# Attention of a routed two-stage MLP kernel: scores from split float32r halves, P*V with V stationary, logits from the transposed output

## What is computed

```python
# attention: q, k, v of shape (B=2, H=8, S=768, D=64); block = 32, window = 16
k_sum = k.reshape(B, H, nb, block, D).max(axis=3)
v_sum = v.reshape(B, H, nb, block, D).mean(axis=3)
scores_l = scale * q @ k.T           # only where abs(i - j) < 16, else -1e9
scores_s = scale * q @ k_sum.T + np.log(block)
a = softmax(concat([scores_l, scores_s]))       # the sum gets 1e-9
x = a @ concat([v, v_sum])           # then 1536 tokens of 512
# experts: E=8, F=1024, tau=0.1
logits = (x / (norm(x) + 1e-6)) @ en.T / tau
out = gate * (np.maximum(x @ w1[e], 0) @ w2[e])  # e = argmax(logits)
# dense: d_ff = 2048
h = out @ w_in
g = (a0 + a1*h + a2*h**2 + a3*h**3) / (1 + abs(b0)*abs(h) + abs(b1)*h**2 + 1e-6)
result = g @ w_out
```

## Time and profile before

| | before |
|---|---|
| time of three runs, median (lowest to highest) | 886.83 us (883.63 to 887.01) |
| span of the profiled execution | 909.4 us |
| the profiled execution's own time outside the span | not given apart |
| PE, PEld busy | 776.2 us (85%), 641.1 us (71%) |
| DVE, ACT, POOL busy | 505.2 us (56%), 410.6 us (45%), 92.5 us (10%) |
| mean granted clock of PE | 0.860 |
| DMA traffic | 80.45 MB, mean 88 GB/s |

### The profile page before, as it was taken

The page is one execution under the profiler, slowest core; times in us unless marked ns, Lnnn a source line. Parts: engine busy times, 40 slices in busy tenths (PEclk is TensorE's granted clock), DMA queues, the critical chain, the costliest instruction groups (busy, mean ns, idle before and its releaser), DMA issues.

```text
span 909.4 us, 13113 instructions
## 1 busy us (share of the span) xinstructions
PE 776.2 (85%) x3557; PEld 641.1 (71%) x3558; DVE 505.2 (56%) x911; ACT 410.6 (45%) x752; POOL 92.5 (10%) x107
## 2 busy tenths in 40 slices
PE   2369999999992198887998998849999989999995
PEld 2268989999992176666876876727778768787884
DVE  4822333335455044655333133148999899989996
ACT  2122222234442153655334244146666666666663
POOL 1120302111002300000000000050000000000000
PEclk9655555569995599999999999968999999999999
DMA  9332131133230454787126125030000100000001
GB/s 209 125 107 58 43 99 43 51 95 92 79 107 35 173 210 172 280 279 271 46 92 254 46 74 180 24 92 12 25 21 3 47 0 0 0 25 22 1 0 47
DMA packets 66388, 80.45 MB, mean 88 GB/s; under 512 B 43568, under 2 KB 43568, under 8 KB 65464
## 3 DMA queue, kind: packets, MB, share of 16 engines
q1 hardware_dynamic: 57224, 54.39, 19.5%
q0 software_dynamic: 6048, 20.45, 6.6%
q10 hardware_dynamic: 3088, 5.26, 1.6%
HBM read 63.48 MB, written 16.61 MB: 88 GB/s over the span
## 4 chain that ended last, share of the span: by engine, by line
PE 54%; DVE 18%; DMA 9%; ACT 8%; issue 5%; SPq 3%; POOL 1%; ACTq 0%; DVEq 0%; POOLq 0%
PE bank L1122 12%; PE bank L949 8%; DMA xg<-x_by_slot 7%; PE bank L1101 6%; PE bank L1009 5%; PE bank L1034 5%; PE bank L1175 5%; PE bank L1190 5%; PE bank L1032 4%; PE bank L1007 3%; DVE qd L905 3%; DVE pb L907 3%; DVE rr L906 3%; ACT rr L604 2%; DVE qd L898 2%
## 5 line engine op out<-in xcount | busy, mean ns | idle before, releaser
L1190 PE MATMUL bank<-weights,G 128*128 128x512 f32 x576 | 144.4, 400 | 6.1 <-DVE G L830 5.9
L1175 PE MATMUL bank<-X2T,weights 128*128 (+1 forms) x576 | 145.8, 403 | 1.6 <-DVE X2T L830 1.6
L1190 PEld LDWEIGHTS bank<-weights,G 128*128 128x128 f32 x576 | 108.9, 190 | 34.2 <-DVE G L830 5.8
L1175 PEld LDWEIGHTS bank<-X2T,weights 128*128 128x128 f32 x576 | 109.9, 192 | 28.6 <-issue 2.4
L1101 PE MATMUL bank<-weights,XT 128*128 (+1 forms) x456 | 116.8, 406 | 5.7 <-DVE XT L830 5.7
L1122 PE MATMUL bank<-weights,HT 128*128 x456 | 118.6, 419 | 2.4 <-DVE HT L830 2.4
L488 ACT ACTIVATE es<-es,nmx 128x182 f32<-128x182 f32 x96 | 42.8, 446 | 146.6 <-DVE nmx L736 146.5
L1122 PEld LDWEIGHTS bank<-weights,HT 128*128 128x128 f32 x456 | 90.0, 200 | 23.9 <-issue 2.6
L1101 PEld LDWEIGHTS bank<-weights,XT 128*128 128x128 f32 x456 | 85.2, 191 | 28.2 <-issue 9.6
L736 DVE CUSTOM_DVE_ANT_0 es<-bank,mask_now 128x182 f32<-128x182 f32 x96 | 33.2, 348 | 127.5 <-PE bank L1009 109.7
L830 DVE TENSOR_TENSOR HT<-bank,HT 128x512 fp32r<-128x512 f32 x38 | 24.5, 686 | 97.3 <-ACT HT L549 97.3
(11 more groups left out here) (167 smaller groups left out, 1188.3 us busy)
## 6 DMA issues: line engine op xcount, KB each, us to landing
raw_early<-in_moe_w_dram SPq DMA_DIRECT2D x14, 1024.0 KB, 5.4
raw_late<-in_moe_w_dram SPq DMA_DIRECT2D x14, 1024.0 KB, 8.8
x_by_slot<-x_all ACTq DMA_DIRECT2D x5, 1024.0 KB, 4.4
xg<-x_by_slot POOLq DMA_DIRECT2D x19, 256.0 KB, 5.5
y_by_slot<-yo POOLq DMA_DIRECT2D x19, 256.0 KB, 2.4
raw_early<-in_moe_w_dram POOLq DMA_DIRECT2D x4, 1024.0 KB, 8.4
kraw<-in_k_dram SPq DMA_DIRECT2D x16, 192.0 KB, 4.5
vraw<-in_v_dram SPq DMA_DIRECT2D x3, 1024.0 KB, 6.8
```

The source lines that it names most:

```text
L1175: last = T_.matmul(bank[6 + f % 2][:, :], W[:, 0, wa, kc * F2 + f * P:kc * F2 + (f + 1) * P], X2T[:, bass.ds(c % 2, 1), xa, kc * C_TOK:(kc ...
L1190: last = T_.matmul(bank[tt][:, :], G[:, f % 2, ga, tt * P:(tt + 1) * P], W[:, 1, wa, f * DM:(f + 1) * DM], start=(f == 0 and n_ == 0), sto ...
```

## The change

All 182-key score matmuls, the products, the logits and the set-up are rewritten; from the norms on, the code is the same but for waits.

- Keys: 16 x 24 = 384 blocks of 32 rows are taken as three groups g of 128 blocks, one block per partition, 1 MB per load (`k_rows`). ACT rounds each to float32r (KHL high), DVE takes the rest (low), PE transposes [high, low] of one row each, 32 per group, four to a bank, and ACT and DVE copy them to KTc (a quarter by DVE). The maximum of a block is a tree of DVE maxima along the free dimension (`key_max`), split and transposed in the same way. V's sums are a tree of additions on POOL (`mean_v`).
- Windows: for each tile POOL copies the 24 maxima and 158 keys of four heads at a time from KTc into KW, float32r (`windows`).
- Queries: POOL splits each query tile into high, low, high (`split_q`); PE transposes [high, low] and [low, high] of each head (`query_stack`, four transposes per pair of heads), and ACT or DVE copies one bank of 512 columns to QS.
- Scores: two float32r matmuls of 182 columns per head into one bank slice. All 128 partitions carry data: high times high plus low times low, then low times high plus high times low.
- Products: V is stationary, 128 columns of two heads; 256 columns of PT (two heads, 128 queries each) move. The diagonal halves are the output, transposed, and are copied to OT by ACT and DVE (`out_half`).
- x: four transposes of OT (`rows_of_x`), scaled into x_all directly (`make_x`). Logits: OT is stationary, 16 columns of EB move; DVE scales and adds over the heads (`make_logits`).
- Everything is written out: 48 units u of one pair of heads, no loop. Query stacks are made two units ahead, transposes run two and products three units behind.
- The first expert's slab is loaded in eight half chunks of 512 KB (from tile 2 on, one per tile) into space of x_all. SP's loads for the next expert wait for the last product.

The core of the diff:

```diff
-                        j = half * 3 + jj
-                        last = transpose(bank[2 * (bp % 2) + half][:, jj * P:(jj + 1) * P],
-                                         kraw[:, j, pr * P:(pr + 1) * P])
+            def key_columns(g):
+                for i in range(g * FILLS, (g + 1) * FILLS):
+                    r0 = i % FILLS * 4
+                    if i % 4 == 0:
+                        pe.wait_ge(k_lo, i // 4 + 1)
+                    if i >= 6:
+                        wait_fills(pe, i - 5)
+                    for r in range(4):
+                        last = transpose(bank[i % 6][:, r * P:(r + 1) * P],
+                                         KHL[:, g % 2, r0 + r, :, :].rearrange("p a d -> p (a d)").bitcast(F32))
...
+            def query_stack(u):
+                T, p = divmod(u, PAIRS)
+                if p == 0:
+                    pe.wait_ge(q_split, T + 1)
+                if u >= 2:
+                    wait_qs(pe, u - 2)
+                if u % 4 == 2 and u >= 10:
+                    pe.wait_ge(x_done, (u - 10) // 4 + 1)
+                if u % 4 == 3 and u >= 11:
+                    pe.wait_ge(lg_read, (u - 11) // 4 + 1)
+                for i in range(2):
+                    row = qhl[:, T % 2, 2 * p + i, :, :].rearrange("p a d -> p (a d)").bitcast(F32)
+                    for swap in range(2):
+                        s = 2 * i + swap
+                        last = transpose(bank[6 + u % 2][:, s * P:(s + 1) * P], row[:, swap * D:swap * D + P])
+                last.then_inc(q_mm, 1)
+
+            def scores(u):
+                T, p = divmod(u, PAIRS)
+                wait_qs(pe, u)
+                if p % 2 == 0:
+                    pe.wait_ge(kw_done, 2 * T + p // 2 + 1)
+                if u >= 2:
+                    pe.wait_ge(s_read, 2 * u - 2)
+                for i in range(2):
+                    for swap in range(2):
+                        last = T_.matmul(bank[u % 2][:, i * 2 * P:i * 2 * P + KEYS], QS[:, u % 4, 2 * i + swap, :],
+                                         KW[:, T % 2, 2 * p + i, :], start=(swap == 0), stop=(swap == 1))
+                    last.then_inc(s_mm, 1)
+
+            def transposes(u):
+                pe.wait_ge(exp_done, 2 * u + 2)
+                if u >= 2:
+                    wait_pt(pe, u - 2)
+                for part in range(2):
+                    for i in range(2):
+                        s = 2 * part + i
+                        last = transpose(bank[2 + u % 2][:, s * P:(s + 1) * P],
+                                         es[:, u % 3, i * KEYS + part * P:i * KEYS + (part + 1) * P])
+                last.then_inc(pt_mm, 1)
+
+            def products(u):
+                T, p = divmod(u, PAIRS)
+                r = T % 2
+                wait_pt(pe, u)
+                if p == 0:
+                    pe.wait_ge(v_in[r], 32 * (T // 2 + 1))
+                    pe.wait_ge(vm_in[r], 16 * (T // TB + 1))
+                if p % 2 == 0 and T >= 1:
+                    wait_ot(pe, 2 * T - 1 + p // 2)
+                O_ = bank[4 + p // 2][:, p % 2 * 2 * P:(p % 2 + 1) * 2 * P]
+                T_.matmul(O_, VA[:, r, p * P:(p + 1) * P], PT[:, u % 2, 0:2 * P], start=True, stop=False)
+                T_.matmul(O_, VB[0:KB, r, p * P:(p + 1) * P], PT[0:KB, u % 2, 2 * P:4 * P], start=False, stop=True)\
+                  .then_inc(pv_mm, 1)
+
+            def rows_of_x(T):
+                wait_ot(pe, 2 * T + 2)
+                if PAIRS * T + 8 < UNITS:
+                    wait_qs(pe, PAIRS * T + 8)
+                if T >= 1:
+                    pe.wait_ge(x_done, T)
+                for p in range(PAIRS):
+                    last = transpose(bank[6][:, p * P:(p + 1) * P], OT[:, T % 2, p, :])
+                last.then_inc(x_mm, 1)
+
+            def logits(T):
+                if PAIRS * T + 9 < UNITS:
+                    wait_qs(pe, PAIRS * T + 9)
+                if T >= 1:
+                    pe.wait_ge(lg_read, T)
+                for p in range(PAIRS):
+                    last = T_.matmul(bank[7][:, p * 2 * E:(p + 1) * 2 * E], OT[:, T % 2, p, :], EB[:, p, :],
+                                     start=True, stop=True)
                 last.then_inc(lg_mm, 1)
...
+            query_stack(0)
+            query_stack(1)
+            for u in range(LOOPS):
+                if u % 4 == 0 and u >= 8:
+                    logits(u // 4 - 2)
+                if u < UNITS:
+                    scores(u)
+                if u + 2 < UNITS:
+                    query_stack(u + 2)
+                if 2 <= u < UNITS + 2:
+                    transposes(u - 2)
+                if 3 <= u < UNITS + 3:
+                    products(u - 3)
+                if u % 4 == 3 and u >= 7 and u // 4 - 1 < NT:
+                    rows_of_x(u // 4 - 1)
```

SP's order of loads, POOL's part, ACT's and DVE's per unit (added lines alone; of SP's order, the query loads, the wait for the cleared tiles and the V row loads stand in unchanged lines between `load_k(1)` and `store_means(0)`):

```diff
+            load_k(0)
+            load_k(1)
+            load_v_all(0)
+            load_v_all(1)
+            load_k(2)
+            store_means(0)
+            load_v_all(2)
+            store_means(1)
...
+            sp.wait_ge(pv_mm, UNITS)
...
+            def split_q(T):
+                r = T % 2
+                pool.wait_ge(q_in[r], 16 * (T // 2 + 1))
+                if T >= 2:
+                    pool.wait_ge(q_mm, PAIRS * (T - 1))
+                G_.tensor_copy(qhl[:, r, :, 0, :], heads(qraw[:, r, :])).then_inc(pool_chain, 1)
+                n[0] += 1
+                G_.tensor_copy(qhl[:, r, :, 2, :], heads(qraw[:, r, :]))
+                pool.wait_ge(pool_chain, n[0])
+                G_.tensor_tensor(qhl[:, r, :, 1, :], heads(qraw[:, r, :]), qhl[:, r, :, 0, :].bitcast(F32),
+                                 ALU.subtract).then_inc(q_split, 1)
+
+            def mean_v(g):
+                pool.wait_ge(v_all_in[g], 16)
+                w = ROW // 2
+                t = vraw[:, g % 2, :]
+                while w >= D:
+                    link(G_.tensor_tensor(t[:, 0:w], t[:, 0:w], t[:, w:2 * w], ALU.add))
+                    w //= 2
+                G_.tensor_scalar(vmean[:, g, :], t[:, 0:D], 1.0 / BLOCK, None, ALU.mult).then_inc(vmean_ready, 1)
+
+            def windows(T, half):
+                b, t, r = T // TB, T % TB, T % 2
+                h0 = 4 * half
+                if T % TB == 0 and half == 0:
+                    wait_fills(pool, (b + 2) * FILLS)
+                    pool.wait_ge(ks_sb, b + 2)
+                if T >= 2:
+                    pool.wait_ge(s_mm, (T - 2) * H + h0 + 4)
+                bh = b * H + h0
+                at = EDGE + bh * S + t * P - HALO
+                G_.tensor_copy(KW[:, r, h0:h0 + 4, 0:NSUM],
+                               KSs[:, bh * NSUM:(bh + 4) * NSUM].rearrange("c (h n) -> c h n", h=4))
+                G_.tensor_copy(KW[:, r, h0:h0 + 4, NSUM:KEYS],
+                               KTc[:, at:at + 4 * S].rearrange("c (h n) -> c h n", h=4)[:, :, 0:LOC])\
+                  .then_inc(kw_done, 1)
...
+            for T in range(2, NT):
+                split_q(T)
+                windows(T, 0)
+                windows(T, 1)
+                if T < 2 * CHUNKS + 1:
+                    split_slab0(T - 1)
...
+            for u in range(LOOPS):
+                if u % 2 == 0 and u + 2 < UNITS:
+                    query_stack(u + 2)
+                if u < UNITS:
+                    exponent(u, 0)
+                if u % 2 == 1 and 2 <= u < UNITS + 2:
+                    copy_pt(u - 2)
+                if u < UNITS:
+                    exponent(u, 1)
+                if u % 4 in (0, 2) and 4 <= u < UNITS + 4:
+                    out_half(u // 4 - 1, u % 4 // 2)
+                if u % 4 == 1 and u >= 9:
+                    square_sum((u - 9) // 4)
...
+            def key_max(g):
+                t = kraw[:, g % 2, :]
+                w = ROW // 2
+                dve.wait_ge(k_lo, 2 * g + 2)
+                link(V.tensor_tensor(t[:, 0:w], t[:, 0:w], t[:, w:2 * w], ALU.max))
+                key_column(g * FILLS + DVE_FILLS[0])
+                while w > 2 * D:
+                    w //= 2
+                    link(V.tensor_tensor(t[:, 0:w], t[:, 0:w], t[:, w:2 * w], ALU.max))
+                key_column(g * FILLS + DVE_FILLS[1])
+                link(V.tensor_tensor(t[:, 0:D], t[:, 0:D], t[:, D:2 * D], ALU.max))
+                link(V.tensor_copy(KMX[:, g, HI, :], t[:, 0:D]))
+                V.tensor_tensor(KMX[:, g, LO, :], t[:, 0:D], KMX[:, g, HI, :].bitcast(F32), ALU.subtract)\
+                 .then_inc(kmax_ready, 1)
...
+            for u in range(LOOPS):
+                if u < UNITS:
+                    if u >= 3:
+                        dve.wait_ge(pt_mm, u - 2)
+                    scored(u, 0)
+                    scored(u, 1)
+                if u % 4 == 0 and u >= 8:
+                    make_logits(u // 4 - 2)
+                if u % 2 == 0 and 2 <= u < UNITS + 2:
+                    copy_pt(u - 2)
+                if u % 2 == 1 and u + 2 < UNITS:
+                    query_stack(u + 2)
```

(6 more changed lines are left out.)

630 lines of the change are left out of this document (296 added, 334 removed).

## The result

The changed kernel takes 857.14 us in the median of four runs (852.64 to 860.77); beside it the kernel before took 883.63 to 936.32 us. The ratio is 0.967, 95% interval 0.961 to 0.974. Timed again in a later session it took 858.86 (855.02 to 864.04) against 880.18 to 945.34. The forecast was 802: right in direction, but 30 us of gain where 85 were forecast. The profiled execution took 860.77 us, of which the span is 859.2.

What follows compares the result with a forecast made beforehand. PE was taken to bound the attention at either clock. Set-up 40.5 + clock start 3 + 12 tiles x 11.2 + 2 = 180 us against 275.3, so span 814 and time 802 (middle of 791 and 814); range 782 to 860.

Steps and rivals of the forecast that it cites:

- What bounds the kernel: Attention: PE is the bound at either clock; a tile took 24.22 us at the low clock, 13.23 at the high.
- First scores at 40.5 (36 to 48): Set-up: key chain on DVE from 11.35 to about 34, then transposes, copy and query stack; first scores at 40.5 us.
- rival 3: Attention: hand-overs or another engine bind, 13.2 us a tile, 826; POOL contending with VectorE, + 44; chance 0.11 together.
- SP's V loads are issued ahead of the block-mean store, so the queue is not held by it.: Set-up, SP queue: the block-mean store would not hold up V loads; PE's V wait goes, keys are late next.
- PE's prices: Attention at the high clock: scores 0.128 us each, products 1.01 a pair, a pair 2.39, a tile 11.2.
- Which clock: Attention: the high clock comes within one or two pairs and stays, 3 us for the start; narrow products and short logits go.
- Other engines, POOL, after attention: Per tile DVE 7.6, ACT 8.6, POOL 7.8 us, hidden under PE's 11.2; after attention 0, at most 2, more.
- The sum: Whole kernel: attention ends at 180 us instead of 275.3, span falls by 95 to 814, time forecast 802.
- The last step, 22.6 us between profiled span and timed median: From span to time: 791 if the 22.6 us carry over, 814 if not; the middle, 802, was taken.
- Slow float32r: Score matmuls: float32r at 182 columns streams no faster than float32, 0.39 us each, + 50 to 852; chance 0.16.
- Low clock throughout: Attention: all 12 tiles at the low clock, 20.5 us each, time 900, slower than before; chance 0.05.
- Hand-overs: Attention: waits between engines for reads and copies keep a tile at 13.2 us, + 24 to 826; chance 0.11 with POOL.

Runs made afterwards that it cites:

- e1_split: Changed kernel with the 89-row V load of each batch's first tile made as two loads, 9 and 80 rows; 832.69 us.
- e3_small: Changed kernel with the four small loads (embedding, coefficients, threshold) issued by SyncE ahead of the keys instead of by ACT beside them; 843.42 us.
- e7_nosum: Changed kernel with GpSimd's tree of V sums left out (block means then wrong); 844.58 us.
- e6_before_split: Kernel before with only the 89-row V load split in two, 9 and 80 rows; 853.02 us, ratio 0.934 to the kernel before.
- e12_single_narrow: Changed kernel with one score matmul a head instead of two and products of 64 columns instead of 256; 939.21 us.
- e9_before_r: Kernel before with KT, KS and QZ as float32r, so its score matmuls run in that type; 931.99 us.

## Why the prediction was right and wrong

**What bounds the kernel.** Right: PE, at either clock; in e1_split PE waits under 1 us at a time for anything from the first scores on.

**First scores at 40.5 (36 to 48).** Wrong, 50.5. Two terms. "The chain starts where today's ends with eT, at 11.35": the small loads went out beside those of keys and V, landed at 11.1, and the chain started at 18.95; ahead of the keys they give 10.26 (e3_small). And the chain of 22.6 us was costed from VectorE rows of stretches in which GpSimd did little; beside its work it took 29.4, without the V sums 25.3 (e7_nosum: 16.32 to 41.59), of which 1.8 are a wait for ScalarE. That is the contention of rival 3, but on VectorE's side and in the set-up. The page it named, "GPSIMD Engine Reference" (1. Specifications) of the Trainium skill, says that the two contend when VectorE reads two SBUF inputs; the runs agree, and give the size: 1.23 to 2.18 us for a maximum of two tiles. They show it too for an instruction with one tile and a scalar column, 0.47 to 2.14. The forecast looked at GpSimd's instruction, which hadn't slowed in the rows, and not at VectorE's. (By its own prices the third low halves would be done at 11.35 + 15 + 2.4 = 28.8, not "near 31"; that made up 2 us.)

**"SP's V loads are issued ahead of the block-mean store, so the queue is not held by it."** The step that failed. The store doesn't hold the queue; the V load itself does, for 13.24 us, and the row for it was there in the kernel before (16.03 us at 41.09, not among the rows the forecast shows). "What is late next is the keys" was wrong for the same reason: it was tile 2's queries, through GpSimd's order. 19.9 us of waits in twelve tiles, more than the 1 us a tile that the forecast gave as a sign of being wrong.

**PE's prices.** Right. Scores 0.133 each (0.128 forecast; the float32 bound of 0.39 is excluded), transposes 0.44 for four, products 1.15 a pair against 1.01: the 256-column matmuls over VB take 0.31 instead of 0.252. Pair 2.55 against 2.39, tile 11.50 (issue to issue of V loads, 105.17 to 116.67) against 11.2. From first scores to last product e1_split takes 138.5 us, the forecast 139.5 (180 - 40.5). That these agree so well is partly luck: twelve tiles cost 3.6 us more, and the 3 us for a low clock at the start weren't needed.

**Which clock.** "I take it that the clock rises in the first one or two pairs and stays": the first half was right, it was up at 47.3, ahead of the first scores. But it fell twice, and 10.4 us were lost to that, behind waits that the forecast didn't have. The reading behind it failed for the long stretch: it explained the low clock by the instructions of the old loop, narrow products and short logits, and left out the wait ahead of them. e6_before_split has the old products at 0.93 to 1.00 in steps of 25 us for 150 us. The wait of 6.50 us in the earlier trace rows, costed at 6.5, was worth 66 in the profiled execution; by the timed medians the repair gave 67 on its own chip and 34 against the 886.83. For the short fall at 234.1 the reading has support: the five others without a wait came behind the same logits, and the changed kernel, without these, has none. Of the rule of the Trainium skill weighed there, that the gate is throttled until the engine's activity releases it, e12_single_narrow says what the kernel before said: PE busy for 10.00 of 10.00 us at 0.50, in all but two of the stretches of 10 us from 80 to 300.

**Other engines, POOL, after attention.** No engine bound the tile. From the last product to the first expert matmul: 40.1 us, as before (40.5). The experts and the dense part, the same code, took 599.8 against 593.6; in the other traces 596.0 to 603.3, with 597.0 and 599.3 behind the old attention (e6_before_split, e9_before_r), so this is no effect of the change.

**The sum.** Last product forecast at 180, measured 219.3: 10.0 (start) + 19.9 (waits) + 10.4 (clock behind them) - 1.0 (PE's work) = 39.3. With -0.4 and +6.2 of the two lines above, 814 becomes 859.1, the measured span being 859.2. The last step, 22.6 us between profiled span and timed median, was the kernel before's own variation and nothing that a profile adds (changed kernel: 860.77 for a span of 859.2). To take half of it off, 12 us, was wrong; of its two ends, 814 was the one to take. These 12, the 39.3 and the 5.8 make up the 55 us between 802 and 857, less 2 between the profiled span and the median.

**The rivals.** Slow float32r: excluded. Low clock throughout: not in this kernel; e12_single_narrow, the new loop without its wide products and its second score matmul, did just that, and took 939.21. Hand-overs: 11.50, not 13.2. The measured time lies inside 782 to 860 by a way that none of them had.

## What to carry to other kernels

Look at the issuing queue's own row before costing anything behind it: an issue of 13 us where its neighbours take 0.4 was a transfer on about one DMA engine, and the odd first tile of a batch was where it stood. A PE wait of 6 to 10 us cost its length and then the clock, about 5 us each in the loop that recovered and 60 in the one that didn't; so ask what stood before the long low stretch began, and not only what instructions it is made of. Before one execution is taken as proof, look how far the same kernel spreads. Price a new chain on VectorE beside GpSimd's new work, not by rows from stretches in which GpSimd did little.
